# Copies issued earlier, value halves spread over a slot, a gather in another order, and fillers: five edits to a fused attention and mixture-of-experts kernel

## The chip, the core and the metric

The kernel runs on one core of a Trainium2 chip. The metric is device time in microseconds (us), the median of several runs. The engines of the core work side by side and meet only at semaphores: TensorE (PE in the rows; its weight loads are PEld), VectorE (DVE), ScalarE (ACT), GpSimd (POOL) and SyncE (SP), which here only issues DMA transfers (its rows carry SPq).

## The reference, cut to what matters

```python
def _attn_ref(q, k, v, centroids):                 # (2, 8, 768, 64), centroids (8, 16, 64)
    q_assign = np.argmax(einsum(q_n, c_n), axis=-1)
    k_assign = np.argmax(einsum(k_n, c_n), axis=-1)
    mask = q_assign[:, :, :, None] == k_assign[:, :, None, :]
    scores = np.where(mask, scale * q @ k.T, -1e9)
    return softmax(scores) @ v
def _moe_ref(x, w_gate, w1, w2):                   # 1536 tokens of 512, 8 experts
    expert_idx = np.argmax(x @ w_gate, axis=1)
    out[mask_e] = gate_w[mask_e] * (relu(x[mask_e] @ w1[e]) @ w2[e])
def _moe2_ref(x, w_in, w_out, alpha):
    h = x @ w_in
    return (max(h, 0) + alpha * min(h, 0)) @ w_out
```

## The kernel before

**Attention.** There are 16 heads, worked on two at a time as 8 pairs j; a head is a slot g = 2j + odd, and `slot` in the tensor program writes TensorE's order by hand. Each operand is held as a high part and a low part, and the products are made from stacked operands: `Q1`, `K1` (112 rows: high part, its first 32 rows again beside the low part, and the clusters' one-hot rows `oh_t`) and `Q2`, `K2` (97 rows). SyncE stacks them by DMA (`stack`, ten copies for a head: `assemble_parts` has four, `assemble_rest` six). The semaphore `s_asm1` counts the six of Q1 and K1, `s_asm2` the four of Q2 and K2. The high parts `Qh`, `Kh` are made by ScalarE (`s_hi`), the low parts `Ql`, `Kl` for pair 0 by VectorE (`s_lo`), `oh_t` by ScalarE (`s_oh`).

In a slot TensorE does: six score tiles (`score_tile`), which ScalarE turns into exponentials; between them, for the next head, six maxima tiles (`max_tile`), each reduced by VectorE to a column of `neg_max` (`s_nm`); and the products with the values of the head before, twelve half tiles (`out_half`, three matmuls each). Behind them stand transposes of the next pair and `max_row`, for which GpSimd makes `diag`. Slot 0 has no head before it; it does head 0's halves 0 to 5 at its end. Slot 1 (`second`) does head 0's halves 6 to 11, all behind its loop over tiles; the later slots do five or six of twelve inside that loop. In slot 0 the maxima alternate between the accumulators `psM` and `psVD`; `out_half` writes `psVD`, so it waits for all maxima. From slot 1 on they use `psM` alone, so each maxima tile waits for the reduction of the last.

**Routing.** When attention ends, tokens are assigned to experts on the chip. `logits` of 12 token tiles; one-hots `roh` on VectorE; `count_tokens` on TensorE; a scan on VectorE (`scan_tiles`), then the one-hot tiles `late_oh` that say which token stands in which place of expert 0, and further steps to the slot numbers `slot_u`. With those GpSimd scatters the rows of X into `xs_slots` in memory. Expert 0's rows are not fetched back: `gather_first` multiplies X by the one-hot tiles, 8 matmuls per token tile (4 chunks of 128 columns, high and low part), into the two banks of `psM` (chunks 0 and 1 in bank 0, 2 and 3 in bank 1). The sum over all 12 tiles must be complete before ScalarE (`xe_hi`, one copy per bank, behind `s_g0` and `s_xp`) and VectorE (`xe_lo`) read a bank. Then `layer1` of expert 0 starts (L1333 on). ScalarE's copies of hidden rows 4 to 7 overwrite X, so they wait for all scatters to land (`s_scat`).

**The rest.** Eight experts, each with two layers of three matmuls per product, and then the dense block `widen`/`narrow`. `keep_warm(n)` issues n matmuls on the identity whose results nobody reads.

## Time and profile before

| | |
|---|---|
| median of 3 runs | 807.01 us (806.98 to 808.05) |
| the profiled execution | 810.97 us |
| its span, the time axis of all rows | 808.6 us |
| TensorE busy | 782.1 us, 97% of the span |
| VectorE / ScalarE / GpSimd busy | 388.6 / 301.5 / 164.5 us |

The page's chain of work that ended last gives 59% of the span to TensorE and 2% to VectorE. Rows of a timeline read: start in us, length in us, engine, line, operation, what is written from what, shape, how many instructions are merged, and in brackets how long the engine had been idle and what ended that. A matmul of 4-byte floats on 128 columns is two instructions, so `x12` of `psVD<-Vp,PT` are six matmuls, two halves. Matmuls overlap: the start of the next row tells the pace, not the row's length.

### The profile page before, as it was taken

The page shows a single profiled execution, that of the slowest core. Times are in us where ns is not written, and L with a number is a line of the kernel's source. Part 1 is how long each engine was busy: PE and PEld are TensorE (multiplying, and loading weights), DVE is VectorE, ACT ScalarE, POOL GpSimd, SP SyncE. Part 2 cuts the span into 40 slices and gives each one's busy share as a digit, 9 for nine tenths or more (in the row PEclk, how much of TensorE's full clock was granted, in tenths as well). Part 3 has the DMA queues.
Part 4 walks back from the last instruction along what each step waited for, and adds up shares of the span by engine and source line. Part 5 has one row for each costly group of instructions (what it writes and reads, how often), then busy time and mean ns, then how long its engine had stood idle before and what let it go on. Part 6 is the DMA issues. An engine that isn't in the chain of part 4 may idle for free.

```text
span 808.6 us, 13269 instructions
## 1 busy us (share of the span) xinstructions
PE 782.1 (97%) x5263; PEld 717.4 (89%) x5263; DVE 388.6 (48%) x640; ACT 301.5 (37%) x454; POOL 164.5 (20%) x163
## 2 busy tenths in 40 slices
PE   7889999999999998999999999999999999999996
PEld 7779999999999998999999999978888888888885
DVE  5725455354554556776666665456250504232230
ACT  4234443444434622546555665445021201211011
POOL 2302212122130003370000000013041403232131
PEclk9999999999999999899999999999999999999999
DMA  6745647566485607478665665331001000000001
GB/s 135 160 98 138 149 102 171 116 151 151 92 239 124 189 1 272 145 200 218 199 202 207 231 231 195 119 144 66 1 1 53 0 1 1 26 27 1 0 14 39
DMA packets 76028, 93.13 MB, mean 115 GB/s; under 512 B 45968, under 2 KB 45968, under 8 KB 75984
## 3 DMA queue, kind: packets, MB, share of 16 engines
q1 hardware_dynamic: 73680, 86.20, 38.5%
q0 software_dynamic: 2304, 6.31, 2.4%
q8 instruction: 32, 0.52, 0.3%
q14 instruction: 12, 0.10, 0.0%
HBM read 59.31 MB, written 12.73 MB: 89 GB/s over the span
## 4 chain that ended last, share of the span: by engine, by line
PE 59%; DVE 2%; ACT 0%; issue 0%; POOL 0%; ACTq 0%; DVEq 0%
PE psS L1431 5%; PE psS L1429 5%; PE psS L1430 5%; PE psS L1348 4%; PE psS L1346 4%; PE psS L1347 4%; PE psVD L1363 4%; PE psVD L1365 4%; PE psVD L1364 4%; PE psVD L1447 3%; PE psM L1447 3%; PE psVD L1446 3%; PE psM L1446 3%; PE psVD L1448 3%; PE psM L1448 3%; DVE w_lo L503 1%
## 5 line engine op out<-in xcount | busy, mean ns | idle before, releaser
L684 PE MATMUL psVD<-Vp,PT 128*128 128x128 f32 x1152 | 150.2, 278 | 1.2 <-DVE neg_max L1049 1.2
L684 PEld LDWEIGHTS psVD<-Vp,PT 128*128 128x128 f32 x1152 | 145.9, 194 | 2.0 <-issue 1.5
L1841 POOL TENSOR_TENSOR g_lo<-gf,g_hi 128x512 fp32r<-128x512 f32 x48 | 62.1, 1293 | 313.7 <-ACT g_hi L1587 313.5
L1049 DVE TENSOR_REDUCE neg_max<-psM 128x1 f32<-128x768 f32 x90 | 86.1, 957 | 63.0 <-PE psM L658 62.6
L503 DVE TENSOR_TENSOR w_lo<-w_raw,w_hi 128x1024 fp32r<-128x1024 f32 x88 | 104.8, 1224 | 21.6 <-ACT w_hi L499 21.0
L1797 DVE TENSOR_SCALAR tmin<-psS,alpha_c 128x512 f32<-128x512 f32 x48 | 36.0, 751 | 149.4 <-PE psS L1431 149.1
L875 ACT ACTIVATE PT<-psS 128x768 f32<-128x768 f32 x96 | 76.9, 812 | 70.6 <-PE psS L676 70.6
L1587 ACT ACTIVATE g_hi<-gf 128x512 fp32r<-128x512 f32 x48 | 30.4, 634 | 163.1 <-DVE gf L1800 163.1
L499 ACT ACTIVATE w_hi<-w_raw 128x1024 fp32r<-128x1024 f32 x88 | 90.5, 1056 | 1.3 <-DMA w_raw<-in_moe_w 1.3
L1346 PE MATMUL psS<-xe_hi,w_hi 128*128 128x224 f32 x284 | 77.9, 274 | 1.4 <-DVE xe_lo L1711 1.4
L1348 PE MATMUL psS<-xe_hi,w_lo 128*128 128x224 f32 x284 | 78.0, 275 | 0.0
L1347 PE MATMUL psS<-xe_lo,w_hi 128*128 128x224 f32 x284 | 77.9, 274 | 0.0
L1363 PE MATMUL psVD<-ht_hi,w_hi 128*128 128x224 f32 x272 | 75.2, 276 | 0.0
L1364 PE MATMUL psVD<-ht_lo,w_hi 128*128 128x224 f32 x272 | 74.6, 274 | 0.0
L1365 PE MATMUL psVD<-ht_hi,w_lo 128*128 128x224 f32 x272 | 74.6, 274 | 0.0
L1431 PE MATMUL psS<-y_hi,w_lo 128*128 128x512 f32 x188 | 74.5, 396 | 0.0
L1429 PE MATMUL psS<-y_hi,w_hi 128*128 128x512 f32 x188 | 74.1, 394 | 0.0
L1430 PE MATMUL psS<-y_lo,w_hi 128*128 128x512 f32 x188 | 73.8, 393 | 0.0
L1168 POOL TENSOR_TENSOR diag<-ident,neg_max 128x384 fp32r<-128x384 f32 x32 | 27.9, 873 | 175.5 <-DVE neg_max L1049 175.5
L673 PE MATMUL psS<-Q,K 112*128 112x384 f32 x192 | 56.1, 373 | 0.3 <-ACT Q L862 0.3
L1346 PEld LDWEIGHTS psS<-xe_hi,w_hi 128*128 128x128 f32 x284 | 54.5, 192 | 1.5 <-DVE w_lo L503 1.5
L1348 PEld LDWEIGHTS psS<-xe_hi,w_lo 128*128 128x128 f32 x284 | 54.5, 192 | 0.0
(267 smaller groups left out, 1451.2 us busy)
## 6 DMA issues: line engine op xcount, KB each, us to landing
w_raw<-in_moe_w SPq DMA_DIRECT2D x18, 2048.0 KB, 10.4
xs_slots<-zero SPq DMA_DIRECT2D x8, 784.0 KB
K<-Kh SPq DMA_DIRECT2D x32, 192.0 KB, 3.0
w_raw<-in_moe_w_in SPq DMA_DIRECT2D x2, 2048.0 KB, 9.1
w_raw<-in_moe_w_out SPq DMA_DIRECT2D x2, 2048.0 KB, 11.1
xe_n<-xs_slots SPq DMA_DIRECT2D x16, 224.0 KB, 8.9
Qn<-in_q SPq DMA_DIRECT2D x16, 192.0 KB, 5.1
Kn<-in_k SPq DMA_DIRECT2D x16, 192.0 KB, 4.0
```

The lines of the kernel that those rows point to most:

```text
L499: nc.scalar.activation(w_hi[slot][:, w], w_raw[slot][:, w], ACT.Copy).then_inc(done, 1)
L503: eng.tensor_tensor(w_lo[slot][:, w], w_raw[slot][:, w], w_hi[slot][:, w].bitcast(F32), ALU.subtract).then_inc(done, 1)
L684: mm = pe.matmul(psV[:, PVS * t:PVS * t + P], PT[par][:, c, t * P:(t + 1) * P], Vp[par][:, c, :], start=(c == 0), stop=(c == T - 1))
L1346: pe.matmul(o, w_hi[slot][:, w], xe_hi[:, c, :], start=(c == 0), stop=False)
L1347: pe.matmul(o, w_hi[slot][:, w], xe_lo[:, c, :], start=False, stop=False)
L1348: mm = pe.matmul(o, w_lo[slot][:, w], xe_hi[:, c, :], start=False, stop=(c == KD - 1))
L1363: pe.matmul(o, w_hi[slot][:, w], h_hi, start=(f == 0), stop=False)
L1364: pe.matmul(o, w_hi[slot][:, w], h_lo, start=False, stop=False)
L1365: mm = pe.matmul(o, w_lo[slot][:, w], h_hi, start=False, stop=(f == FT1 - 1))
L1429: pe.matmul(o, w_hi[2 - 2 * a][:, w], y_hi[:, c, :], start=(c == 0), stop=False)
L1430: pe.matmul(o, w_hi[2 - 2 * a][:, w], y_lo[:, c, cols], start=False, stop=False)
L1431: mm = pe.matmul(o, w_lo[2 - 2 * a][:, w], y_hi[:, c, :], start=False, stop=(c == KD - 1))
```

## The change

Five edits, none to what is computed.

1. SyncE, start: the ten stacked copies of head 0 are issued in another order. The five that need only high parts go as soon as `s_hi` is there; the others wait each for its own source.
2. Slot 1: halves 6, 7 and 8 of head 0 move into the loop over tiles, behind the maxima of tiles 1, 2 and 3; halves 9, 10 and 11 stand one by one where two stood.
3. Slot 0: five filler matmuls between the last exponential and the wait for the maxima, into bank 0 of `psS`.
4. Routing: the count of tokens stands inside the gather of the fifth tile (number 4), behind its first four matmuls; and six filler matmuls stand behind the gather of tile 5.
5. Routing: the gather of the late tiles 6 to 11 goes over all tiles for bank 0, then over all tiles for bank 1. `s_g0` is now raised half way instead of four matmuls from the end.

```diff
 WARM0, WARM1, WARM2, WARM3 = 10, 8, 2, 3
+WARM4, WARM5 = 6, 5
             sp.wait_ge(s_hi, 2)
+            stack(Q1[0], 0, D, Qh, 0, s_asm1[0])
+            stack(K1[0], 0, D, Kh, 0, s_asm1[0])
+            stack(Q1[0], D, 96, Qh, 0, s_asm1[0])
+            stack(Q2[0], D, 96, Qh, D // 2, s_asm2[0])
+            stack(K2[0], 0, D, Kh, 0, s_asm2[0])
             sp.wait_ge(s_lo, 1)
-            assemble_parts(0)
+            stack(K1[0], D, 96, Kl, 0, s_asm1[0])
             sp.wait_ge(s_oh, 1)
+            stack(Q1[0], 96, 112, oh_t, 0, s_asm1[0])
+            stack(K1[0], 96, 112, oh_t, 64, s_asm1[0])
+            stack(K2[0], D, 96, Kl, D // 2, s_asm2[0])
             sp.wait_ge(s_lo, 2)
-            assemble_rest(0)
+            stack(Q2[0], 0, D, Ql, 0, s_asm2[0])
             assemble_parts(1)
             assemble_rest(1)
...
+                    if second and 2 <= t < 5:
+                        out_half(0, t + 4)
...
                     pe.wait_ge(s_v[0], 16)
                     pe.wait_ge(s_exp, T)
+                    keep_warm(WARM5, 0)
                     pe.wait_ge(s_nm, 2 * T)
                     out_half(0, 0)
                     out_half(0, 1)
-                if prev:
+                if second:
+                    out_half(0, 9)
+                elif prev:
                     out_half(1 - odd, 6)
                     out_half(1 - odd, 7)
...
             gather_first(pe, 3)
-            gather_first(pe, 4)
+            gather_first(pe, 4, range(2))
             count_tokens(pe, NT, EARLY_STEPS + 4)
-            for u in range(T - 1, NT - 1):
-                gather_first(pe, u)
-            gather_first(pe, NT - 1, range(2)).then_inc(s_g0, 1)
-            gather_first(pe, NT - 1, range(2, KD)).then_inc(s_xp, 1)
+            gather_first(pe, 4, range(2, KD))
+            gather_first(pe, 5)
+            for _ in range(WARM4):
+                pe.matmul(psS[:, 3, 0:P], ident[:, :], ident[:, :], start=True, stop=True)
+
+            for u in range(T, NT):
+                mm = gather_first(pe, u, range(2))
+            mm.then_inc(s_g0, 1)
+            for u in range(T, NT):
+                mm = gather_first(pe, u, range(2, KD))
+            mm.then_inc(s_xp, 1)
```

SyncE's order at the start, head 0's ten copies, of before (`Q_0_88` is Q1 of head 0, `K_0_92` K1, `Q_0_90` Q2, `K_0_94` K2):

```order
L523 DMA Q_0_88<-Qh 64x768
L523 DMA K_0_92<-Kh 64x768
L523 DMA Q_0_88<-Qh 32x768
L523 DMA K_0_92<-Kl 32x768
L523 DMA Q_0_88<-oh_t 16x768
L523 DMA K_0_92<-oh_t 16x768
L523 DMA Q_0_90<-Ql 64x768
L523 DMA Q_0_90<-Qh 32x768
L523 DMA K_0_94<-Kh 64x768
L523 DMA K_0_94<-Kl 32x768
```

and the same place of the change:

```order
L524 DMA Q_0_88<-Qh 64x768
L524 DMA K_0_92<-Kh 64x768
L524 DMA Q_0_88<-Qh 32x768
L524 DMA Q_0_90<-Qh 32x768
L524 DMA K_0_94<-Kh 64x768
L524 DMA K_0_92<-Kl 32x768
L524 DMA Q_0_88<-oh_t 16x768
L524 DMA K_0_92<-oh_t 16x768
L524 DMA K_0_94<-Kl 32x768
L524 DMA Q_0_90<-Ql 64x768
```

The sixth copy for Q1 and K1, which raises `s_asm1` to what TensorE waits for, is K1's from `oh_t` in both; two copies for Q2 and K2 now stand ahead of it.

TensorE's order from the fifth score tile of slot 1 to its end, of before (`x6` are six matmuls, two halves):

```order
L673 MATMUL psS<-Q_1_89,K_1_93 128x384 x2
L676 MATMUL psS<-Q_1_91,K_1_95 128x384 x2
L658 MATMUL psM<-K_0_92,Q_0_88 128x384 x2
L673 MATMUL psS<-Q_1_89,K_1_93 128x384 x2
L676 MATMUL psS<-Q_1_91,K_1_95 128x384 x2
L658 MATMUL psM<-K_0_92,Q_0_88 128x384 x4
L684 MATMUL psVD<-Vp_78,PT_96 128x128 x6
L612 MATMUL psM<-ident,Qn 128x128 x6
L684 MATMUL psVD<-Vp_78,PT_96 128x128 x6
L665 MATMUL psM<-diag,ones_r 128x384 x2
L684 MATMUL psVD<-Vp_78,PT_96 128x128 x6
L612 MATMUL psM<-ident,Kn 128x128 x6
```

and of the change:

```order
L682 MATMUL psS<-Q_1_89,K_1_93 128x384 x2
L685 MATMUL psS<-Q_1_91,K_1_95 128x384 x2
L667 MATMUL psM<-K_0_92,Q_0_88 128x384 x2
L693 MATMUL psVD<-Vp_78,PT_96 128x128 x3
L682 MATMUL psS<-Q_1_89,K_1_93 128x384 x2
L685 MATMUL psS<-Q_1_91,K_1_95 128x384 x2
L667 MATMUL psM<-K_0_92,Q_0_88 128x384 x4
L693 MATMUL psVD<-Vp_78,PT_96 128x128 x3
L621 MATMUL psM<-ident,Qn 128x128 x6
L693 MATMUL psVD<-Vp_78,PT_96 128x128 x3
L674 MATMUL psM<-diag,ones_r 128x384 x2
L693 MATMUL psVD<-Vp_78,PT_96 128x128 x3
```

A half now stands behind each of three maxima tiles (one of them in this piece), and one half instead of two stands ahead of the transposes, ahead of `max_row` and behind it.

## Rows read from the trace of the kernel before

**Rows 1.** The page: the span, and TensorE's busy time.

```profile
span 808.6 us, 13269 instructions
...
PE 782.1 (97%) x5263; PEld 717.4 (89%) x5263; DVE 388.6 (48%) x640; ACT 301.5 (37%) x454; POOL 164.5 (20%) x163
```

**Rows 2.** Busy time by stretch; behind POOL the granted clock, DMA share, GB/s.

```profile
37.50:40.80 3.30, 3.30 (x16) 3.30 (x17) 0.00 (x0) 0.00 (x0) 0.71 (x1) 0.50 0.50 102
...
54.50:57.90 3.40, 3.40 (x18) 3.40 (x17) 0.96 (x1) 0.00 (x0) 0.98 (x2) 0.50 0.80 174
...
320.80:327.50 6.70, 6.00 (x28) 6.00 (x29) 5.98 (x29) 0.00 (x0) 1.45 (x2) 0.50 0.55 218
```

**Rows 3.** Timeline of TensorE, from the start into slot 1.

```profile
17.93 0.61 PE L693 MATMUL psS<-ident 128*128 128x128 f32 x4
20.49 0.58 PE L658 MATMUL psM<-K,Q 112*128 112x384 f32 x2 [1.95 <-DMA K<-oh_t]
...
37.45 2.90 PE L684 MATMUL psVD<-Vp,PT 128*128 128x128 f32 x12 [1.20 <-DVE neg_max L1049]
...
42.93 1.50 PE L684 MATMUL psVD<-Vp,PT 128*128 128x128 f32 x12
44.19 0.60 PE L673 MATMUL psS<-Q,K 112*128 112x384 f32 x2
```

**Rows 4.** Timeline of TensorE, end of slot 1.

```profile
52.40 0.62 PE L658 MATMUL psM<-K,Q 112*128 112x384 f32 x2 [0.43 <-DVE neg_max L1049]
54.06 0.67 PE L658 MATMUL psM<-K,Q 112*128 112x384 f32 x2 [1.05 <-DVE neg_max L1049]
54.53 2.76 PE L684 MATMUL psVD<-Vp,PT 128*128 128x128 f32 x12
...
61.75 0.60 PE L673 MATMUL psS<-Q,K 112*128 112x384 f32 x2
```

**Rows 5.** Timeline of TensorE, routing: count, gather, first layer, second expert.

```profile
317.30 0.39 PE L403 MATMUL psVD<-roh,ones 128*128 128x96 f32 x2
...
318.33 0.27 PE L426 MATMUL psM<-early_oh,early_x_lo 128*128 128x224 f32 x1
...
321.50 0.56 PE L425 MATMUL psM<-late_oh,late_x_hi 128*128 128x224 f32 x1 [2.90 <-DVE late_oh L491]
...
329.71 0.27 PE L426 MATMUL psM<-late_oh,late_x_lo 128*128 128x224 f32 x1
...
354.63 0.34 PE L1346 MATMUL psS<-xe_hi,w_hi 128*128 128x224 f32 x1 [1.38 <-DVE xe_lo L1711]
```

**Rows 6.** Timeline of VectorE, routing: one-hots, scan, slot numbers.

```profile
316.52 0.21 DVE L465 TENSOR_TENSOR roh<-ex_prio,rmax 128x48 f32<-128x48 f32 x1
319.15 0.26 DVE L475 COPY scan<-psVD 128x96 f32<-128x96 f32 x1 [2.42 <-PE psVD L403]
```

**Rows 7.** Timeline of SyncE's queue, start.

```profile
9.40 1.34 SPq L516 DMA_DIRECT2D Kn<-in_k  x2
14.64 0.54 SPq L523 DMA_DIRECT2D Q<-Qh  x1
...
18.25 0.59 SPq L523 DMA_DIRECT2D K<-oh_t  x1
```

**Rows 8.** Timeline of ScalarE, start.

```profile
9.58 0.83 ACT L884 ACTIVATE Kh<-KTr 128x768 fp32r<-128x768 f32 x1
14.74 0.99 ACT L857 ACTIVATE oh_t<-psM,sw_bias,sw_scale 128x768 fp32r<-128x768 f32 x1 [4.33 <-PE psM L651]
```

**Rows 9.** Timeline of VectorE, start and slot 1.

```profile
30.43 0.56 DVE L972 CAST Qh<-QTr 128x768 fp32r<-128x768 f32 x1 [1.15 <-DMA K<-Kl]
...
54.77 0.96 DVE L1049 TENSOR_REDUCE neg_max<-psM 128x1 f32<-128x768 f32 x1 [0.76 <-PE psM L658]
```

**Rows 10.** Timeline of SyncE's queue: first fetch that waits for all scatters.

```profile
335.81 1.76 SPq L1238 DMA_DIRECT2D xe_n<-xs_slots  x4
```

**Rows 11.** Timeline of ScalarE, first hidden rows that overwrite X.

```profile
337.85 0.36 ACT L1478 ACTIVATE ht_hi<-psS 128x224 fp32r<-128x224 f32 x1 [1.00 <-PE psS L1348]
```

More of the change, by code:

```diff
@@ L686, in out_half, with keep_warm @@
                 return mm
-            def keep_warm(n):
+            def keep_warm(n, bank=3):
                 for _ in range(n):
-                    pe.matmul(psS[:, 3, 0:P], ident[:, :], ident[:, :], start=True, stop=True)
+                    pe.matmul(psS[:, bank, 0:P], ident[:, :], ident[:, :], start=True, stop=True)
             pe.wait_ge(s_const, 1)
@@ L796, in slot @@
                     out_half(0, 3)
-                if prev:
+                if second:
+                    out_half(0, 10)
+                elif prev:
                     out_half(1 - odd, 8)
@@ L810, in slot @@
                     out_half(0, 5)
-                if prev:
+                if second:
+                    out_half(0, 11).then_inc(s_pv, 1)
+                elif prev:
                     out_half(1 - odd, 10)
```

## The prediction

> **What bounds the kernel now.** I read the page first: TensorE is busy 782.1 of 808.6 us [rows 1], so time can only come out of the 26 us in which it stands still, or of stretches in which it runs at half clock; busy time does not show the latter. So I read the granted clock by stretch next. It is 0.50 of full speed, 1.2 instead of 2.4 GHz, in 37.50 to 40.80, in 54.50 to 57.90 and in 320.80 to 327.50, with TensorE busy 3.30, 3.40 and 6.00 us [rows 2]. At full clock that work takes half, so each of the first two costs about 1.7 us and the third 3.0. Then I read TensorE's timeline for what was ahead of each fall. Ahead of the first it stood still for 1.20 us, waiting for the maxima [rows 3]; ahead of the second for 0.43 and 1.05, again for maxima [rows 4]; ahead of the third for 2.90, waiting for `late_oh` [rows 5]. Last, who is late: at the start it is the last stacked copy, TensorE idle 1.95 us until 20.49 [rows 3]; in routing it is the count's release, the scan and VectorE up to the second expert [rows 5, 6]. Between slot 2 and routing, and behind the second expert, the order is not touched and TensorE is the bound, so whatever is won ahead of those parts arrives at the end whole. The sum is made on the profiled execution, span 808.6 and own time 810.97; the runs without profile have a median of 807.01, 4.0 below, and I take the same difference off both.
>
> **Edit 1, the early copies.** SyncE issues one copy per 0.6 us. Now it begins at 14.64, and K1's copy from `oh_t` goes at 18.25 [rows 7]; TensorE starts on the maxima at 20.49 [rows 3], 2.24 behind it. SyncE is free from 9.40 + 1.34 = 10.74 [rows 7] and `Kh` is done at 9.58 + 0.83 = 10.41 [rows 8]. Five copies from 10.8 take till 14.0. K1's from `Kl` stays where the first copy was, 14.64. `oh_t` is done at 14.74 + 0.99 = 15.73 [rows 8], so the two from it go at 15.8 and 16.4, and the last lands at about 16.4 + 2.24 = 18.6. TensorE's fillers end at 17.93 + 0.61 = 18.54 [rows 3], just ahead. Gain 18.25 - 16.4 = **1.85**. It is bounded from below by the DMA queues: five copies now follow at once on the load of pair 1. If those slow each other, the last one lands later; I keep 1.0 as the lower end. Little more than 1.85 is possible, since fillers and dots hold TensorE until 18.5. In slot 0, VectorE also waited 1.15 us at 30.43 for the last copy of head 1 [rows 9], 20 copies from 14.64. Now 14 follow from 15.8, so that copy comes about 3 us earlier and the wait is gone. The maxima behind it are held by TensorE's own score tiles, so I count 0.2 more at the wait for all maxima (0 to 0.4).
>
> **Edit 3, fillers in slot 0.** Two rows of matmuls on 128 columns are one filler. Twelve such rows take 44.19 - 42.93 = 1.26 us [rows 3], so ten take 1.1. The last exponential is done by when the last maxima tile is, and the idle stretch behind that tile is 1.20 [rows 3], so the fillers fit into it and cost nothing; if the wait for maxima shrinks by 0.4, they cost 0.3. What they give is the clock: with TensorE busy up to 37.45 instead of idle, the value halves and transposes run at full clock. Gain **1.7** (0 if the clock falls all the same).
>
> **Edit 2, halves in slot 1.** Slot 1 takes 61.75 - 44.19 = 17.6 us [rows 3, 4]. Its loop goes by maxima: a reduction takes 0.96 [rows 9], a maxima tile 0.4 and the handing over the rest, and from 52.40 to 54.06 is one round, 1.66 [rows 4]. A half is 1.26 / 2 = 0.63 us. In a round of the new order TensorE has maxima 0.36, half 0.65, score 0.72, so 1.73: three rounds grow by 0.1 or less each, and the last maxima tile comes at 54.2 instead of 54.06. Behind it, now: two halves and transposes to 58.15 at half clock, `max_row`, two halves, transposes, next slot at 61.75. New, walked through by its waits: half 9 to 55.2; transposes when the last maximum is there, 54.9 + 0.96 = 55.9, to 56.5; half 10 to 57.2; ScalarE's copy of the transposes done at 57.65, `max_row` to 58.05; half 11 to 58.7; ScalarE's row of maxima at 59.2; transposes, next slot at 59.9. Gain 61.75 - 59.9 = **1.85** if the clock holds. The waits of VectorE and ScalarE fill this end now, so at half clock most of the slower work hides in them: I price a fall at 1.1.
>
> **Edits 4 and 5, routing.** Three things move.
> The count: four matmuls fewer stand ahead of it. The one-hots are done at 316.52 + 0.21 = 316.73 [rows 6], the count can start there instead of at 317.10, and VectorE's scan, all later VectorE steps, and the scatters move by 0.25. The scan starts at 319.15 though the last count matmul's row ends at 317.69 [rows 5, 6], 1.46 us in which the rows show no other cause. I keep this lag as it is.
> The fillers: twelve rows, 1.3 us. Gather and fillers last until 318.60 + 1.3 = 319.9; the idle time ahead of the late gather falls from 2.90 to 1.3, and TensorE is busy through most of what was idle. The late gather's 48 matmuls took 321.50 to 329.99 [rows 5]; at the early gather's pace of 0.11 each they take 5.4, from 321.25 to 326.7, 3.3 earlier.
> The banks: ScalarE copies bank 0 while TensorE sums bank 1, so one copy of 0.5 and half the subtraction come off the path; VectorE is busy with slot numbers until about 327.2 all the same. First layer: 3.5 earlier.
> But this does not arrive whole. SyncE's fetch at 335.81 [rows 10] is the moment in which the last scatter has landed. ScalarE's hidden row 4 needs that too and came at 337.85, waiting for TensorE [rows 11]: a slack of 2.0 us. Scatters come only 0.25 earlier, at 335.55, the first layer 3.5. So ScalarE stops until 335.55; behind it come four hidden rows and three weight copies of 1.05 between them, the last hidden row ends at about 339.8 instead of 342.15, and VectorE's chain behind it moves by 2.4. That chain is what TensorE waits for at 354.63, 1.38 us [rows 5]; that wait will grow to about 2.4. Routing gives **2.4**, with 1.9 and 3.6 as ends.
>
> **Sum.** 1.85 + 0.2 + 1.7 + 1.85 + 2.4 = 8.0. Span 808.6 - 8.0 = 800.6, profiled execution 803.0, median 807.0 - 8.0 = **799.0**.
>
> **Rivals.**
> - *The clock falls once more, at the end of slot 1.* For: four short waits (1.3, 0.65, 0.5, 0.5) stand in the new order between 52.9 and 59.3, and before, 0.43 and 1.05 were enough [rows 4]. Against: at the start 1.95 idle us did not bring it down [rows 3], and TensorE works between these. Time: 799.0 + 1.1 = 800.1, chance 0.14. The Trainium skill, page "TensorE: Matmul & The Clock Gate", section "Part 4: PE-mode transpose", says that transposes do not count as busy for the clock in the way matmuls do. By it the six transposes there would not help and the fall would come, so the time would be 800.1. No row of before settles it: no transposes stand ahead of either fall.
> - *A filler does not hold the clock.* In slot 0 that takes 1.7 back, 800.7. In routing, late gather at half clock ends near 329.7, only the overlap of the banks is left, and routing gives 0.6 instead of 2.4: 800.8. Against: the idle time ahead is less than half of what it was. Chance 0.08 together.
> - *The count's release waits for TensorE to run empty.* For: the scan came 0.55 after the last row of the gather behind the count, 318.33 + 0.27, not after the count [rows 5, 6]. Against: nothing else in the rows works so. Then twelve fillers and four more matmuls push it to about 320.4, 1.3 later than before; scatters too, the stop at ScalarE grows, and routing gives 0.8: 800.6. Chance 0.08.
> - *The lag of 1.46 is gone.* Then scatters land at 334.1, the stop vanishes and routing gives 3.6: 797.8. Chance 0.12.
> - *Slower than before: the scatters land late.* Place: ScalarE's wait ahead of hidden row 4. Each us by which they land behind 337.85 delays all that follows by as much. The other edits give 5.6, so it turns at 337.85 + 5.6 = 343.4, 7.6 behind the 335.81 of now; at 345 the time is 808.6. The DMA engines are busy with weights there, yet nothing in the change adds to their work. Chance 0.03.
> - *No measurable change*: gains at the start are taken back in the loop over pairs. TensorE waits for so little there that I see no place for it. Chance 0.02.
>
> **Numbers.** The forecast holds 0.53: 797.9 to 800.2 by its own terms. A kernel like this tells 0.2%, 1.6 us, from no change: 805.4 to 808.6. All cases but the last two are below: faster 0.95, same 0.02, slower 0.03. The range reaches down to the lag gone with 1 us to spare, and up to a clock fall with the early copies at their lower end, 800.8 + 0.85: 796.8 to 801.6.
>
> **What would show it.** First maxima tile at 18.6 (right) or past 19.4 (copies slow each other). Clock 1.00 from the start through slot 2, next slot at 56.1 on the new time axis; a granted 0.50 in 30 to 60 shows an edit of the clock wrong. In routing, from the last logits on: the late gather with rows 0.11 apart; from the count's last row to the scan about 1.5; ScalarE's hidden row 4 ended by DMA, not by TensorE; the wait ahead of the second expert near 2.4. Wrong it is above all if the clock falls somewhere else, or if a wait of 1 us opens in the loop over pairs.

## The result, and the profile after

The kernel after took 803.02 us (median of 4 runs, 802.03 to 804.09), the kernel before 807.53 beside it (4 runs, 806.98 to 808.35): ratio 0.9934, 95% interval 0.9916 to 0.9952, which stays below 1. It is faster, by 4.5 us where 8.0 were forecast, and outside the range, which ended at 801.6. In a later comparison on another chip it was 803.81 (12 runs) against 807.18 (35 runs), ratio 0.9957 [0.9936, 0.9978].

The page of the kernel after, its first part:

```profile
span 801.7 us, 13317 instructions
...
PE 780.0 (97%) x5285; PEld 715.4 (89%) x5285; DVE 389.1 (49%) x640; ACT 301.0 (38%) x454; POOL 163.7 (20%) x163
```

The profiled execution has a span of 801.7 against 808.6 [rows 1], and a time of 804.09 against 810.97: 6.9 less, not 4.5. The difference between these two numbers is the main finding below. A *fall* is from here on a stretch in which the granted clock is 0.50, 1.2 instead of 2.4 GHz; every trace has one more at its end, with no matmul in it; that one is not counted.

Busy time by stretch of the kernel after (behind POOL the granted clock, DMA share, GB/s):

```profile
30.00:62.00 32.00, 28.95 (x196) 26.07 (x196) 14.35 (x19) 14.88 (x19) 8.74 (x9) 1.00 0.51 112
347.70:351.00 3.30, 3.30 (x17) 3.30 (x17) 0.78 (x2) 1.13 (x3) 2.44 (x3) 0.50 0.99 328
```

The three falls of [rows 2] are gone. A new one stands at 347.6, behind the wait for the second expert, and takes 1.6 us back.

SyncE's queue: the first early copy, and the sixth of the six for Q1 and K1, for which TensorE waits:

```profile
10.97 0.65 SPq L524 DMA_DIRECT2D Q<-Qh  x1
...
16.10 0.59 SPq L524 DMA_DIRECT2D K<-oh_t  x1
```

TensorE's timeline, start to slot 2, and the second expert:

```profile
19.84 0.59 PE L667 MATMUL psM<-K,Q 112*128 112x384 f32 x2 [1.52 <-DMA K<-oh_t]
...
35.41 1.28 PE L702 MATMUL psS<-ident 128*128 128x128 f32 x10
36.69 1.60 PE L693 MATMUL psVD<-Vp,PT 128*128 128x128 f32 x12
...
41.82 0.60 PE L682 MATMUL psS<-Q,K 112*128 112x384 f32 x2
...
51.83 0.62 PE L667 MATMUL psM<-K,Q 112*128 112x384 f32 x2 [1.05 <-DVE neg_max L1067]
...
57.57 0.59 PE L682 MATMUL psS<-Q,K 112*128 112x384 f32 x2
...
315.76 0.35 PE L426 MATMUL psM<-late_oh,late_x_hi 128*128 128x224 f32 x1
...
321.08 0.28 PE L427 MATMUL psM<-late_oh,late_x_lo 128*128 128x224 f32 x1
...
346.10 0.34 PE L1371 MATMUL psS<-xe_hi,w_hi 128*128 128x224 f32 x1 [1.78 <-DVE xe_lo L1736]
```

The copy from `oh_t` is issued at 16.10 instead of 18.25 [rows 7], but TensorE starts on the maxima at 19.84 instead of 20.49 [rows 3]: of 2.15 us at the issue, 0.65 arrive. The fillers (35.41) fill the wait at the end of slot 0. Slot 1 takes 57.57 - 41.82 = 15.75 us instead of 17.6 [rows 3, 4]. The late gather takes 321.36 - 315.76 = 5.6 instead of 8.5 [rows 5], since its clock holds. The second expert starts 8.5 us earlier than in [rows 5]; 1.6 of that go in the new fall. Stage by stage, from one profiled execution to the other: the start 0.65, the end of slot 0 1.7 (28.78 to 44.19, now 28.14 to 41.82), slot 1 1.8, and from the end of the last logits to the second expert 4.4 (39.15, now 34.79).

VectorE, ScalarE and SyncE in the routing:

```profile
312.35 0.21 DVE L466 TENSOR_TENSOR roh<-ex_prio,rmax 128x48 f32<-128x48 f32 x1
313.39 0.26 DVE L476 COPY scan<-psVD 128x96 f32<-128x96 f32 x1 [0.83 <-PE psVD L404]
...
321.51 0.21 DVE L1695 TENSOR_TENSOR reached<-ramp_o,bfirst 128x48 f32<-128x48 f32 x1
321.75 1.15 DVE L1736 TENSOR_TENSOR xe_lo<-psM,xe_hi 128x448 fp32r<-128x448 f32 x2
```

```profile
329.67 0.36 ACT L1503 ACTIVATE ht_hi<-psS 128x224 fp32r<-128x224 f32 x1 [1.75 <-DMA xs_slots<-X,slot_u]
```

```profile
329.66 1.93 SPq L1256 DMA_DIRECT2D xe_n<-xs_slots  x4
```

The scan starts 1.04 us behind `roh`; before, that was 2.63 [rows 6]. ScalarE's hidden row 4 now waits for the scatters, not for TensorE as in [rows 11], and starts in the moment in which SyncE's fetch is let go: the gate that the forecast put there.

### The profile page after: what moved, and what is told of

Its sections match the earlier page's. It is cut to its first block, busy times and chain, and to the rows that moved or that the text cites. A ratio compares the mean times of both kernels' runs of the same rounds, so it can differ in the third digit from the quotient of the medians.

```text
span 801.7 us, 13317 instructions
## 1 busy us (share of the span) xinstructions
PE 780.0 (97%) x5285; PEld 715.4 (89%) x5285; DVE 389.1 (49%) x640; ACT 301.0 (38%) x454; POOL 163.7 (20%) x163
## 4 chain that ended last, share of the span: by engine, by line
PE 56%; DVE 2%; POOL 2%; issue 1%; ACT 1%; DMA 0%; POOLq 0%; ACTq 0%
PE psS L1456 5%; PE psS L1454 5%; PE psS L1455 5%; PE psS L1373 4%; PE psS L1372 4%; PE psS L1371 4%; PE psVD L1388 4%; PE psVD L1390 4%; PE psVD L1389 4%; PE psVD L1472 3%; PE psM L1472 3%; PE psVD L1471 3%; PE psM L1471 3%; PE psVD L1473 3%; PE psM L1473 3%; POOL xs_slots L1837 1%
## 5 line engine op out<-in xcount | busy, mean ns | idle before, releaser
L693 PE MATMUL psVD<-Vp,PT 128*128 128x128 f32 x1152 | 148.1, 275 | 0.0
L693 PEld LDWEIGHTS psVD<-Vp,PT 128*128 128x128 f32 x1152 | 143.9, 191 | 0.8 <-DVE neg_max L1067 0.2
L1372 PEld LDWEIGHTS psS<-xe_lo,w_hi 128*128 128x128 f32 x284 | 55.3, 195 | 0.0
```

What stands on the lines that cost most here:

```text
L693: mm = pe.matmul(psV[:, PVS * t:PVS * t + P], PT[par][:, c, t * P:(t + 1) * P], Vp[par][:, c, :], start=(c == 0), stop=(c == T - 1))
L1372: pe.matmul(o, w_hi[slot][:, w], xe_lo[:, c, :], start=False, stop=False)
```

## The experiments

Each run also gives the mean granted clock over its span, and with many runs of one kernel that is a view of its own. Some of the runs on the chip of section 1 (before has 35, after 12):

| before: mean clock | us | after: mean clock | us |
|---|---|---|---|
| 0.998 (5 runs) | 803.7 to 804.4 | 0.998 (3 runs) | 802.4 to 802.5 |
| 0.993 to 0.994 (11 runs) | 806.8 to 808.5 | 0.995 to 0.996 (5 runs) | 803.1 to 803.9 |
| 0.989 to 0.990 (8 runs) | 809.2 to 811.1 | 0.994 (2 runs) | 805.9, 806.1 |
| | | 0.992 (2 runs) | 807.1, 807.3 |

For the 35 runs of before the straight line has 0.65 us per 0.001 of clock, correlation -0.94. A fall in the traces is 3.4 us long as a rule (the one at 320.7 was twice that, and one beside a wait of 18.7 us in section 6 was 20.5); 3.4 us at 0.50 take 0.002 off the mean clock of 806 us, by the line 1.4 us. So it is mostly the number of falls that an execution catches that spreads one and the same kernel over 7 us. The trace of before had three within its work and was, with 810.97, near the slow end of its own runs.

### 1. The two kernels again

> The kernel before, unchanged, for the spread of its own executions. Theory A (the price of the clock): the profiled execution of before held 10.2 us at a granted clock of 0.5, its unprofiled ones fewer, so the runs here differ by 1.5 to 4 us and the longer ones have the lower mean clock, 0.990 against 0.994 to 0.998. Theory B (the change itself gives less than its profile shows): all runs have the mean clock of the profile, 0.990, within 0.001, and their times do not follow it. Ratio 1.000 by both.

> The changed kernel, unchanged, for a narrower interval and its own spread. Theory A: ratio 0.992 to 0.995, times 801.5 to 804.5, the longer runs with the lower mean clock (0.996 against 0.998). Theory B: the same ratio, but the runs of before and of this stand apart by the same amount at every clock.

Measured: before unchanged 807.06 (804.28 to 809.79, 12 runs), ratio 0.9999 [0.9976, 1.0022] to its own kind. After 803.81 (802.36 to 807.27), ratio 0.9957 [0.9936, 0.9978]. The new trace of before has falls at 37.6 and 54.6 and none at 320. The new trace of after has three, at 54.0, 347.5 and 528.4. Its windows:

```profile
54.10:57.30 3.20, 3.20 (x16) 3.20 (x15) 0.00 (x0) 0.81 (x1) 0.68 (x2) 0.50 0.78 175
347.60:350.80 3.20, 3.20 (x17) 3.20 (x17) 0.42 (x2) 0.36 (x1) 2.29 (x4) 0.50 0.89 216
528.50:531.80 3.30, 3.30 (x9) 2.52 (x10) 3.29 (x6) 3.30 (x6) 0.00 (x0) 0.50 0.02 5
```

What follows: which falls a trace holds is a draw. The runs of before did spread with the mean clock as theory A had it (its 10.2 us at 0.50 in the first trace were in fact 13.6). The spans of the two traces are 805.5 and 804.9, and a comparison of those alone would say that the change gives 0.6.

### 2. The parts alone

The start alone (edit 1 in the kernel before):

```diff
-            assemble_parts(0)   # before: all ten copies behind s_lo
+            stack(Q1[0], 0, D, Qh, 0, s_asm1[0])
+            ...                 # the order of edit 1
```

> Before with edit 1 alone, the early copies. As predicted, 1.85 us and more: first maxima tile at 18.6, time 2.0 less. Theory Q (the copies queue behind each other in the DMA engines, so the last one takes 3.6 us to land instead of 2.1): first maxima tile at 19.8, 0.65 us less on the path. The clock may add or take up to 2 us by itself.

The routing alone (edits 4 and 5 in the kernel before):

> Before with edits 4 and 5 alone. As predicted 2.4 less. From the changed kernel's profile: second expert 4.4 us nearer to the last logits. Theory A: 4.4 against an execution of before with the fall in routing, 1.5 to 3 against one without it. If the lag of the count's release is the cause of the surplus, the profile shows the scan within 0.1 us of the count's last matmul.

Measured: start 807.11 (803.28 to 809.07, 12 runs), ratio 0.9992 [0.9971, 1.0013]; routing 807.97 (805.96 to 809.78, 12 runs), ratio 1.0005 [0.9985, 1.0025]. Neither can be told from no change by its time. The trace of the start alone is a lucky draw, free of falls until the last matmul, with a span of 801.7, as short as that of the whole change. Its last copy was issued at 16.49 and landed at 19.99, 3.5 us later, as theory Q has it; the maxima start at 20.12, 0.4 earlier than in [rows 3], where the forecast had 1.9. Behind that it is the old slots at full clock (TensorE's timeline):

```profile
20.12 0.59 PE L666 MATMUL psM<-K,Q 112*128 112x384 f32 x2 [1.58 <-DMA K<-oh_t]
...
37.08 1.58 PE L692 MATMUL psVD<-Vp,PT 128*128 128x128 f32 x12 [1.20 <-DVE neg_max L1057]
...
44.02 0.62 PE L666 MATMUL psM<-K,Q 112*128 112x384 f32 x2 [0.16 <-DMA K<-oh_t]
...
52.50 0.62 PE L666 MATMUL psM<-K,Q 112*128 112x384 f32 x2 [1.05 <-DVE neg_max L1057]
```

The same 1.20 us of idle time stands at 37.08 as in [rows 3], and the matmuls behind it run at full pace (1.58 for twelve, not 2.90). An idle stretch ahead of work permits a fall; it doesn't fix one. The trace of the routing alone had falls at 23.0, 53.8, 350.7 and 531.6. In it the scan comes 0.14 us behind the count, and from the end of the last logits to the second expert it takes 34.8 us, against 35.6 in the trace of before without a fall there (section 1): 0.8 less, where the forecast had 2.4 and theory A 1.5 to 3.

### 3. Fillers in every idle place of the kernel before

Five behind the last exponential of slot 0, four ahead of slot 1's last maxima tile, ten behind gather 5, six ahead of the second expert, six ahead of the dense block, and nothing else.

> Before with nothing but filler matmuls in the five places where TensorE stands still for over 1 us: slot 0's end (5), ahead of slot 1's last maxima tile (4), ahead of the late gather (10), ahead of the second expert (6), ahead of the dense block (6). Theory A (clock falls, differing from execution to execution, are what spreads the runs of before, and the changed kernel's gain is mostly fewer of them): no or few falls, mean clock 0.997 to 0.998 in nearly all runs, median 804.0 to 804.6, that is 2.5 to 3 us below before and within 1 us of the changed kernel. Theory B (the moved work gives the gain, fillers do not): median within 1 us of before.

Measured: 805.81 (804.57 to 806.15, 6 runs) beside 808.88 (806.85 to 811.29, 17 runs), ratio 0.9955 [0.9939, 0.9971], with one fall left, at 22.5. Fillers alone, and none of the other edits, are worth about as much as the whole change, and the spread shrinks from 4.4 us (17 runs) to 1.6 (6 runs). Theory B is out; theory A had the clock nearly right (0.995 to 0.999) but the median 1.2 to 1.8 us too low, for two groups of fillers cost time. The ten behind gather 5 are too many: the late gather starts 2.82 behind the scan, instead of 2.35. And the dense block starts 1.0 us later behind the start of the second expert than in the traces without fillers or falls there (179.9 instead of 178.9 us; section 4 shows how). And with ten fillers behind the count the scan came 0.09 us behind it, so the rival by which the count's release waits for TensorE to run empty is out.

### 4. All of it

The kernel after, with the six copies for Q1 and K1 first in the start's order (those for Q2 and K2 behind them), and fillers at the three places where falls were left:

```diff
+            for _ in range(4): ...   # slot 1, ahead of the last maxima tile
+            for _ in range(6): ...   # ahead of the second expert
+            for _ in range(6): ...   # ahead of the dense block
```

> The changed kernel with a third order of the early copies (all six for Q1 and K1 first) and with fillers also ahead of slot 1's last maxima tile (4), the second expert (6) and the dense block (6). Theory A: mean clock 0.998, median 801.0 to 801.6, which is the changed kernel's own full-clock time, 802.4, less up to 1.2 for the copies, and a spread under 1.5 us. Theory B: 803 to 804, spread as before.

Measured: 802.79 (802.25 to 803.82, 6 runs), ratio 0.9919 [0.9904, 0.9934], the lowest ratio of all, though its interval still meets that of the kernel after (0.9916 to 0.9952); all six runs lie within 1.6 us. The median is neither theory's. Its trace has no fall but the one behind the last matmul. TensorE ahead of the second expert:

```profile
346.07 0.34 PE L1375 MATMUL psS<-xe_hi,w_hi 128*128 128x224 f32 x1 [0.42 <-DVE xe_lo L1745]
```

The wait is 0.42 instead of 1.78, and the second expert starts when it did in the kernel after (346.10): these fillers cost nothing. Those ahead of the dense block do (TensorE's timeline):

```profile
525.11 1.58 PE L1486 MATMUL psS<-ident 128*128 128x128 f32 x12 [1.84 <-issue]
526.44 0.48 PE L1446 MATMUL psS<-y_hi,w_hi 128*128 128x512 f32 x1
```

TensorE stands still for 1.84 us ahead of them, with nothing in the profile that it waits for ("issue"), and the dense block comes behind them: 3.17 us behind the last matmul of the experts, instead of the 1.75 in which it waits for ScalarE without fillers. That is 1.4 us lost here, 1.0 in section 3 and 0.9 in section 8; a fall in the dense block costs 1.55. The clock held in all three traces although TensorE had stood still for 1.4 to 1.8 us, so it is not a filled wait that kept it up there, if it was the fillers at all. Why the fillers start late is open; without the 1.4 us the median would have been in theory A's range (an estimate: 801.4).

The other order of copies gave nothing: the last one was issued at 16.55 and landed at 19.68, the first maxima tile came at 19.82.

### 5. The bank order, and the count, by themselves

The kernel after with the late gather tile by tile again:

```diff
-            for u in range(T, NT):
-                mm = gather_first(pe, u, range(2))
-            mm.then_inc(s_g0, 1)
-            for u in range(T, NT):
-                mm = gather_first(pe, u, range(2, KD))
+            for u in range(T, NT - 1):
+                gather_first(pe, u)
+            gather_first(pe, NT - 1, range(2)).then_inc(s_g0, 1)
+            mm = gather_first(pe, NT - 1, range(2, KD))
             mm.then_inc(s_xp, 1)
```

> The changed kernel with the late gather in the old order, tile by tile, its other edits kept. As predicted, the order by banks takes one copy of 0.5 us and half a subtraction off the path: here the first layer is 0.8 later. Theory O (the second bank's copy and subtraction end the path in both orders, and the old order already hid the first bank's): from the last late matmul to the end of the first hidden tile 2.08 us as before, the second expert unmoved within 0.1 us, times as the changed kernel's at the same clock.

Measured: 803.92 (801.75 to 804.26, 6 runs), ratio 0.9926 [0.9908, 0.9943], no different from the kernel after, as theory O has it. Its ScalarE and VectorE behind the late gather:

```profile
321.17 0.99 ACT L1496 ACTIVATE xe_hi<-psM 128x448 fp32r<-128x448 f32 x2 [8.83 <-PE psM L427]
```

```profile
321.74 0.21 DVE L1693 TENSOR_TENSOR reached<-ramp_o,bfirst 128x48 f32<-128x48 f32 x1
321.98 1.16 DVE L1734 TENSOR_TENSOR xe_lo<-psM,xe_hi 128x448 fp32r<-128x448 f32 x2
```

ScalarE copies both banks in one go at 321.17, where the kernel after had copied bank 0 at 318.72. But `xe_lo` follows directly on VectorE's chain of slot numbers, without a wait, in both kernels (321.51 + 0.21 to 321.75 above; 321.74 + 0.21 to 321.98 here). From the gather's last matmul to the end of the first hidden tile it is 2.08 us with the bank order and 2.09 without. From the end of the last logits to the second expert it is 34.79 in both. Edit 5 gives nothing.

The count alone, moved into the fifth gather of the kernel before:

> Before with the count alone moved, inside the gather of tile 4. Theory L (moving the count is the whole gain of routing at full clock): from the last logits to the scan 2.1 us instead of 2.85, second expert 0.75 nearer to the logits. Rival: the count gives the 0.25 by which it starts earlier, and the rest of the changed kernel's 0.75 comes from the fillers or the banks; then 2.6.

Measured: 808.13 (806.57 to 810.31, 12 runs), ratio 0.999 [0.9977, 1.0003]. The scan came 0.09 us behind the count and 2.08 behind the last logits, 0.8 earlier than in the traces of before with the lag, as theory L has it; sections 3 and 8 have the old place without the lag, and there it is 2.30. Its trace has falls at 22.0, 39.1, 349.7 and 530.6, and none at 320, without a filler in the routing.

### 6. What holds the early copies

The kernel after with a sixth of the second pair's query and key rows loaded; the rest of the tiles keeps the first pair's rows, so heads 2 and 3 and all that follows from them are computed from wrong rows (847.57 us in the one run; later the trace goes another way, with a wait of 18.7 us for weights in the experts, and only its start is read):

```diff
-            load_qk(1)
+            for par in range(2):
+                sp.dma_start(Qn[:, 0:1, par * D:(par + 1) * D], qd[2 + par][:, 0:1]).then_inc(s_qn, 16)
+            ...                 # the same for Kn
```

> The changed kernel with a sixth of the second pair's query and key rows loaded (the first of the six row groups of each; the other five keep what the first pair left there, so heads 2 and 3 are computed from the wrong rows). It takes about 0.64 MB out of the transfers that lie between the issue at 8.3 us and the landing at 14.9 us, and changes nothing in SyncE's order of issue. Theory A (the early copies are held by full DMA engines: issued at 16.10, the last copy landed at 19.71, 3.6 us, where the same copy of the kernel before took 2.1 us at a DMA share of 0.12): the last copy lands 2.0 to 2.3 us after its issue, the first maxima tile begins at 18.2 to 18.8 us, and the span is 1 to 1.6 us shorter than with the full loads at the same number of clock falls. Theory B (the copies wait for each other on their queue, or for SyncE's slow slots of issue, whatever else moves): landing and maxima tile stay within 0.3 us of 19.7 and 19.84.

Measured: the sixth copy is issued at 16.12 and has landed at 18.49, and TensorE:

```profile
18.62 0.58 PE L670 MATMUL psM<-K,Q 112*128 112x384 f32 x2 [0.28 <-DMA K<-oh_t]
```

Busy time by stretch, DMA share next to last, of the kernel before while its sixth copy was under way (18.25 to 20.35),

```profile
18.00:20.00 2.00, 0.54 (x5) 0.35 (x4) 0.00 (x0) 0.64 (x2) 0.00 (x0) 1.00 0.62 131
```

of the kernel after,

```profile
10.00:12.00 2.00, 2.00 (x20) 2.00 (x19) 1.83 (x7) 0.59 (x1) 0.00 (x0) 1.00 1.03 233
12.00:14.00 2.00, 1.21 (x11) 1.02 (x10) 1.90 (x5) 0.00 (x0) 0.00 (x0) 1.00 1.10 255
14.00:16.00 2.00, 1.91 (x16) 1.46 (x14) 1.78 (x3) 1.47 (x2) 0.00 (x0) 1.00 1.01 224
16.00:18.00 2.00, 1.73 (x15) 1.73 (x16) 0.83 (x2) 1.98 (x3) 0.00 (x0) 1.00 0.69 153
18.00:20.00 2.00, 0.48 (x4) 0.32 (x4) 0.00 (x0) 0.43 (x2) 0.00 (x0) 1.00 0.50 111
```

and with the small load:

```profile
10.00:12.00 2.00, 2.00 (x20) 2.00 (x20) 1.83 (x7) 0.36 (x1) 0.00 (x0) 1.00 0.37 82
...
14.00:16.00 2.00, 1.74 (x16) 1.50 (x14) 1.78 (x3) 1.45 (x2) 0.00 (x0) 1.00 0.90 194
16.00:18.00 2.00, 1.70 (x15) 1.71 (x16) 0.85 (x2) 1.98 (x3) 0.00 (x0) 1.00 0.29 51
```

With most of the load out of the way the maxima start at the forecast's 18.6, to 0.02; the two terms of that sum are each off by 0.3 and cancel (issued at 16.12, forecast 16.4; 2.50 behind it, forecast 2.24), which is luck. What holds edit 1 is the traffic ahead: from 10 to 16 us the DMA engines are full with the second pair's rows and the early copies. The sixth copy takes 3.6 us from issue to landing, against 2.4 here, and against 2.1 in the kernel before, whose copies began when the load had landed (13.74). It is so in every trace: 2.10 or 2.11 in the seven with the old start, 3.1 to 3.7 in the six with the new start and the full load. (The recorded share of 0.12 for before is that of 14 to 16 us; the share under way was 0.62, as above.)

The mean share does not tell how: while the slow copy is under way it is 0.69 and 0.50, no higher than in the kernel before. The semaphore's counts tell more. TensorE waits for 96, 16 for each of the six copies. In the kernel after 94 of them are in at 18.41, 2.3 us behind the issue; the last two come at 19.54 and 19.71. With the small load all 96 are in at 18.49. So here nearly everything had landed about as fast as before, and a small part came late; in the other five traces with the new start 94 counts are in 2.5 to 3.4 us behind the issue. That the late part stood behind older transfers fits with the effect of the load; the runs do not show it.

The Trainium skill, page "DMA: Bandwidth & Descriptors", section "Anatomy of one DMA — SWDGE (gpsimd) path", gives for a transfer that GpSimd issues about 2.0 us plus the bytes over 436 GB/s, by which these 48 KB would take an estimated 2.1 us. These copies are issued by SyncE, for which the section gives no sum; the traces with the old start have the same 2.1. The 3.6 us of the kernel after are not in that sum, which knows one transfer alone.

### 7. Without the fillers

The kernel after with `WARM4, WARM5 = 0, 0`:

> The changed kernel with both groups of fillers set to none (five at the end of slot 0, six behind gather 5). Theory A (the fillers keep the clock up in slot 0, and the falls come in some executions and not in others): a fall returns in slot 0, at 36 to 38 us, in most executions, none in the late gather, where TensorE's idle time is short without them too once the count is moved; the median is 804.5 to 806, the fastest execution is 802.0 to 802.6 as with the fillers, and the spread is wider than that of the run with all fillers (1.6 us). Theory B (the fillers are idle ballast: the falls come at random, whatever TensorE does in those gaps): the median lies within 0.5 us of the changed kernel's 803.8.

Measured: 806.22 (802.44 to 807.93, 10 runs) beside 807.93, ratio 0.9967 [0.9949, 0.9985]. The fastest run is as fast as with fillers. The median is 2.4 us above the 803.8 of section 1, but that was another chip: the two ratios, 0.9967 and 0.9957, have intervals that overlap widely, in the means both kernels are 2.9 to 3.0 us below the kernel before beside them, and the spreads are 5.5 us (10 runs) and 4.9 (12 runs). By their time these eleven fillers can't be told from none; what speaks for them is the count of falls below. As theory A has it, none came in the late gather, where TensorE's idle stretch is short once the count is moved. The trace has falls at 348.8 and 529.7, and the one of slot 0 is back, at 38.2 (TensorE's timeline; the same row took 1.60 with fillers ahead of it):

```profile
37.48 2.29 PE L693 MATMUL psVD<-Vp,PT 128*128 128x128 f32 x12 [1.20 <-DVE neg_max L1067]
```

### 8. The slots alone, and a leaner version

Edits 2 and 3 in the kernel before:

> The kernel before with the value halves of head 0 spread over slot 1 and the five fillers at the end of slot 0, nothing else of the change. Theory A (at full clock the parts add up: 0.5 for the early copies, 0.6 for the halves, 0.8 for the count): at full clock throughout 803.4 us, slot 1's part 15.7 us, the scatters' slot numbers 1.47 or 0.66 us behind the count as before; the median is 805 to 806.5, since the falls of the routing, of the second expert and of the dense block stay. Theory B (the forecast's slot term of 1.85 us holds apart from falls): 802.2 at full clock and a median under 805.

Measured: 805.58 (802.77 to 807.58, 10 runs) beside 807.93 (806.75 to 810.94, 21 runs), ratio 0.9964 [0.9947, 0.998]; the only run at a mean clock of 0.998 took 802.8, between the 803.4 of theory A and the 802.2 of B; the median is in A's range. The trace has falls at 21.6 and 55.7, and no lag behind the count (0.09), which neither theory had.

Edits 2 and 3, the count in the gather, and fillers in five places, with the old start and the old banks:

> The kernel before with the halves of head 0 spread over slot 1, the count inside the fifth gather, and fillers in five idle places (slot 0, before slot 1's last maxima, behind gather 5, before the second expert, before the dense block); the old order of the first copies and the old order of the late gather. Theory A (the bank order gives nothing, the early copies about 0.5 us): median 803.2 to 803.6, with a spread under 2.5 us. Theory B (the early copies give nothing that remains): 802.8 as the fastest version so far. Theory C (the bank order or the copies are what the fillers build on): over 804.5.

Measured: 804.81 (804.29 to 805.26, 6 runs), ratio 0.9954 [0.9939, 0.9969]: theory C's number, over 804.5, with less than A's spread (1.0 us). Of C's two causes the bank order is out by section 5. It is 2.0 above the version of section 4 (on another chip), which has the new start. TensorE's start shows where:

```profile
21.05 0.59 PE L659 MATMUL psM<-K,Q 112*128 112x384 f32 x2 [2.23 <-DMA K<-oh_t]
...
23.57 0.99 PE L659 MATMUL psS<-K,Q 112*128 112x384 f32 x2
```

The maxima begin at 21.05 and not at 19.82, and then the clock falls, at 23.0: a maxima tile takes 0.99 instead of 0.59, and the maxima phase up to slot 0 takes 8.94 instead of 8.29. That is 1.9 us; the two profiled spans differ by 1.5, since the fillers ahead of the dense block cost 0.5 less here.

## Why the prediction was right in sign and wrong in size

**The step that failed is the last one of the sum: "I take the same difference off both".** The 4.0 us between the profiled execution of before and the median of its runs were taken for a constant. They were mostly falls. The time of the profiled execution is its span plus 2.4 us in both kernels, falls or not, and from run to run the time goes with the mean clock (table above). So the three falls in [rows 2], 1.7, 1.7 and 3.0 us, were priced in the 8.0 as if every execution had them, while the number that the sum was taken off, 807.01, is by the line above one with a mean clock of 0.994 and not 0.990. Measured against its own kind the sum fares better: from one profiled execution to the other the span fell by 6.9, and by 8.5 up to the new fall at 347.6, where 8.0 was forecast. That near hit is in part luck: the start gave 0.65 for 1.85 and 0.2, the routing 4.4 for 2.4.

How often the falls come, in all 14 traces of the study ("of" is the number of traces with that form of the place):

| place | without filler or edit | with |
|---|---|---|
| maxima ahead of slot 0 (edit 1) | 5 of 7 | 0 of 7 |
| end of slot 0 (fillers) | 4 of 6 | 0 of 8 |
| end of slot 1 (edit 2; then fillers) | 3 of 5 old order, 2 of 6 new order | 0 of 3 |
| late gather (fillers) | 1 of 6 | 0 of 8 |
| ahead of the second expert (fillers) | 6 of 11 | 0 of 3 |
| ahead of the dense block (fillers) | 5 of 11 | 0 of 3 |

Only the first two lines are unlikely to be chance. One fall in six against none in eight tells nothing of the fillers ahead of the late gather, and three traces are few for the last two lines. At the start the idle stretch ahead tells the two apart: 0.28 to 1.95 us where the clock held, 2.18 to 2.59 where it fell. The big fall at 320.7, the longest and most of the routing's 2.4, came once in 14 traces. The two last places were not in the forecast at all, though "if the clock falls somewhere else" stood there as what would make it wrong. They are as old as the kernel before; the trace of the count alone, with the old start and slots, has both.

**What the change gives at full clock.** From the runs at a mean clock of 0.998 in section 1, 804.0 to 802.4: 1.6 us; over all clocks the 12 runs of the change lie 1.9 below the line through the 35 of before. From the traces, stage by stage, rows without a fall in them:

| stage | old form | new form | gain |
|---|---|---|---|
| start of the maxima (edit 1) | 20.3 to 21.2 (7 traces) | 19.8 to 20.5 (6 traces) | 0.7 in the mean |
| slot 1 to slot 2 (edit 2) | 15.93 and, with a wait for the copies of the second pair, 16.36 | 15.74 | 0.2 to 0.6 |
| logits' end to count's end (edit 4) | 2.21 | 1.99 | 0.22 |
| count's end to scan (edit 4) | 1.47, 0.66, 0.64, 0.09, 0.09 | 0.09 to 0.14 (9 traces) | 0 to 1.4 |
| late gather to first hidden tile (edit 5) | 2.09 | 2.08 | 0 |

The rest is falls that come less often. In the runs of section 1 the mean clock rose from 0.9937 to 0.9954, which by 0.65 us per 0.001 is 1.1; with the 1.9 that is 3.0, the whole difference of their means (807.30 and 804.32). In the four runs of the result it was 0.9968, by the same line 2.0, so 3.6 to 3.9 of the 4.5 us are accounted for.

**Point by point.**
- *Edit 1, 1.85, at least 1.0:* mis-sized, 0.65 in the pair of traces. The issue came as early as worked out (16.10, forecast 16.4), the 2.24 us behind it did not hold (3.74). The bound "from below by the DMA queues" was named and then set too high, without working out how full the engines would be: the second pair's rows are four transfers of 192 KB, the first five copies three of 192 and two of 96, together 1.57 MB, and at the 233 to 255 GB/s of the rows above that is 6.2 to 6.8 us from 10 us on. That the order of section 4, with 0.3 MB of it behind, landed no earlier is not fully explained: its second pair's rows landed at 15.98 instead of 14.93. Not foreseen is that with the shorter wait the clock stays up in the maxima (0.67 us where it falls). Both together are 1.23 + 0.65 of the 2.0 us by which section 8's lean version is behind.
- *Edit 1, 0.2 more in slot 0:* gone. The row before slot 0's value halves waits 1.20 with the new start as with the old.
- *Edit 3, 1.7:* the mechanism is right (fillers fit, no fall in 8 traces); the term holds in an execution with that fall (1.7), and 4 of 6 had one.
- *Edit 2, 1.85:* the new order's length was right to 0.05 (15.7 forecast, 15.75 measured). Its counterpart was mis-sized: the 17.6 us of [rows 3, 4] held a fall, and at full clock the old order takes 15.93, so 1.6 of the 1.85 were that fall. The loop goes by six rounds of reductions on VectorE in both orders: the last maxima tile starts 9.88 us into the slot in the old one (section 5, the count alone) and 10.01 in the new. Behind it the old order takes 6.05 without a wait, the new one 5.73 with waits of 0.47, 0.31 and 0.23: of three halves, 1.9 us of matmuls, that moved away from the end, 0.3 arrive.
- *The rival of a fall at the end of slot 1:* it came in 2 of 6 traces, and cost 1.0 (slot 1 16.70 and 16.75, not 15.74), forecast 1.1. That in one execution six transposes stood behind the idle stretch and the clock held (the kernel after, 53.6), and in another it fell at 54.0, in the same order, leaves open the rule of the Trainium skill, page "TensorE: Matmul & The Clock Gate", section "Part 4: PE-mode transpose", by which transposes do not count as busy in the way matmuls do.
- *Edits 4 and 5, 2.4:* in the pair of traces 4.4, more than the rival of the vanished lag gave (3.6). The gate at the scatters was right, and so was the pace of the late gather (5.6, forecast 5.4). But without a fall in the old late gather it takes 5.62 there too, and the gate lies at the scatters in both kernels: from the start of the scan to the second expert the new trace of before takes 32.70 us, the kernel after 32.71. So at full clock the routing is worth what the count is worth, 0.2 and the lag. (The forecast's 0.25 for the count came out, though its own start times, 317.10 and 316.73, would have given 0.37.) The forecast idle time of 2.4 ahead of the second expert was 1.78.
- *The lag behind the count:* it vanished, as the rival with 0.12 said. It is not TensorE running empty (section 3). It is not the count's place alone either, for two traces with the old place had none. Three of five against none of nine may still be a link; the runs don't settle it.

Faster, at 0.95, was right, and by mechanisms the forecast had; by size it was the forecast of one execution, not of the median. The interval "by its own terms", 797.9 to 800.2, was narrower than those terms: their ends added give 797.6 to 800.6.

## What to carry to other kernels

Before you price a stretch at half clock, look at how the runs without a profile spread and where the profiled one stands among them: if it is at the slow end, its falls are not the median's, and a sum over them has to be weighted by how often each comes. Fillers alone, in five places, gave as much here as the four reorderings without them (0.9955 and 0.9967), with a smaller spread. But they are not free by themselves: in four places they fitted into the wait, ten where six would do cost 0.5 us, and ahead of the dense block they started late and cost 0.9 to 1.4, nearly what the fall there costs. Look in the trace at when the work behind them starts. A transfer that is issued earlier lands earlier only if the DMA engines have room: add the bytes already under way before you move the issue time through to the landing.

## What the runs showed of the hardware

- The granted clock fell or held with the same idle stretch ahead: 1.20 us at the end of slot 0 (4 falls of 6), 1.75 to 1.78 ahead of the second expert and the dense block (6 and 5 of 11, one of these behind 3.48 in section 6). At the start it held behind 0.28 to 1.95 us (9 traces) and fell behind 2.18 to 2.59 (5 traces). A fall was 3.4 us long, the one at 320.7 was 6.8, and one beside a wait of 18.7 us was 20.5 (section 6).
- A fall cost 0.67 us in the maxima, 1.6 at the end of slot 0, 1.6 to 1.7 at the end of slot 1 in the old order and 1.0 in the new, 1.6 in the second expert and 1.55 in the dense block.
- A copy of 48 KB took 2.1 us from issue to landing when the load ahead of it had landed 4.5 us before, at a DMA share of 0.62, and 3.6 behind six microseconds at a share of 1.0 to 1.1, with all but two of the 96 counts in 2.3 us behind its issue. One of SyncE's issues (at 17.36, the copy from `Ql`) took 1.44 us instead of 0.6 behind it.
- The release of a semaphore by a matmul came 0.09 to 0.14 us behind the row's end in eleven traces, and 0.64, 0.66 and 1.47 in three, with a DMA share of 1.0 in all fourteen. The cause is open.
